# Attention with top-32 and a feed-forward block on one core: early queries and keys loaded ahead into idle tiles

## The chip, the cores and the metric

The kernel runs on one core of one Trainium2 chip. The metric is the device time of one execution in microseconds (us). Three executions of the kernel before took 791.53, 792.13 and 792.80 us; the median is 792.13 us.

## The reference

```python
# q, k, v: [4, 8, 576, 64] f32; w_in [512, 2048]; w_out [2048, 512]
scores = (q @ k^T) / 8
kth    = np.partition(scores, -32, axis=-1)[..., -32]       # 32nd largest of each row
scores = np.where(scores >= kth, scores, -1e9)
attn   = exp(scores - max) / (sum + 1e-9)
x      = (attn @ v), heads laid side by side -> [2304, 512]
h      = x @ w_in
g      = h * tanh(softplus(h))                              # mish
y      = g @ w_out                                          # [2304, 512]
```

## The kernel before

**Tiling.** Two heads are a pair, so a batch has four pairs (`PPB`), and the keys of four pairs are held at a time in `k_hi` and `k_lo`. The work runs in 72 duos. A duo `s` is two score tiles of 128 queries by 576 keys. Four duos make a block of 128 rows of `x`, so there are 18 blocks, and each block goes on through the feed-forward part. The first four duos use pairs 0, 1, 2 and 3 in turn.

**Precision.** The score product is made from three passes of reduced-precision matmuls. Keys and queries are split into a high half, written by ScalarE (ACT) as a copy (`split_k` L405, `split_q` L412), and a low half, written by GpSimd (POOL) as raw minus high (L560, L566). `w_out` is split in the same way in eight chunks (ACT L416, POOL L571).

**Stages of a duo.** TensorE (PE) makes the scores (L298) in the one PSUM buffer `ps_s`. ACT copies them to `x_sb` (L423). VectorE (DVE) finds the top 32 of each row with four MAX8 and three MATCH_REPLACE8 (L533, L540, L548). POOL takes the threshold and the negated maximum from it (`negate`, L587 and L589), ACT makes a penalty (L431), POOL subtracts it (`exponents`, L596), ACT exponentiates with a row sum (L439), POOL adds 1e-9 to the sum (`guard`, L600), DVE inverts it (`inverse`, L523), POOL multiplies (`normalise`, L607), PE transposes (L316), ACT copies (L448), PE multiplies by the values (L341 and L334). Blocks then go through `up` (L357), Mish, and `down` (L370).

**Order.** Each engine has one program written out by hand, and it works in that order; loads are issued by SyncE (SP) in its own order. At step `s` of the loop ACT does, in order: copy of the transposed tile of `s-3`, penalties of `s-1`, query split of `s+3`, feed-forward copies, score copies of `s+2`, exponentials of `s-1`, key splits due at `s`, `w_out` splits due at `s` (chunks 0 and 1 at step 0). POOL does at step `s`: `negate(s-1)`, the feed-forward split, `w_out` low parts due at `s-1` (chunks 0 and 1 at step 1), `normalise(s-2)`, `exponents(s-1)`, low query part of `s+3`, `guard(s-1)`, low key parts due at `s`. The key splits of pairs 2 and 3 are due at steps -1 and 0. DVE does `topk(s)` for one duo after another. In `topk(s)` the first MAX8 waits for `negmax_ready` of duo `s-2`, since there are two lists (`LISTS = 2`); and after the first pair of MATCH_REPLACE8 it does `inverse(s-2)`, which waits for `guard(s-2)`.

**Raw tiles.** `k_raw` has two places and `q_raw` one. SP therefore waits, before the query load of duo `s`, for the low query part of duo `s-1` (L219), and before the key load of pair `g` for the low part of pair `g-2` (L213). SP's order before the loop is: keys 0, queries 0, keys 1, `w_out` chunks 0 and 1, queries 1, keys 2, keys 3, four value loads, queries 2, four loads of `w_in` of 1 MB each; queries 3 come first in the loop. `y_sb` is written for the first time by the feed-forward output at step 15, and the third place of `p_sb` by the penalties of duo 2.

Of the kernel before, what the change touches and what calls it, by code (L numbers as in the profile page):

```python
# [5 lines left out]
F32 = mybir.dt.float32  # L6
F32R = mybir.dt.float32r
ALU = mybir.AluOpType
ACT = mybir.ActivationFunctionType

P = 128
# [4 lines left out]
PAIRS, PPB = B * H // 2, H // 2  # L16
# [12 lines left out]
DUOS = BLOCKS * PPB  # L29
# [5 lines left out]
RAWS, QS = 2, 2  # L35
XS, PS_, TS, LISTS = 4, 3, 4, 2
# [32 lines left out]
def q_cols(s):  # L69
    return 2 * P if is_mixed(s // PPB) else P  # L70


FIRST_USE, LAST_USE = {}, {}
# [26 lines left out]
                _uses.append((_g, _w, _s, _s))  # L100


def w_chunks_at(s):
    return [c for c in range(WCHUNKS) if max(c - 1, 0) == s]

# [5 lines left out]
def program(nc, k_in, q_in, v, w_in, w_out, y_out):  # L111
    with ExitStack() as ctx:
# [6 lines left out]
        def sem(name):  # L119
            return ctx.enter_context(nc.semaphore(name))  # L120

        k_raw = sb("k_raw", [P, RAWS, S])
        k_hi = sb("k_hi", [P, PPB, S], F32R)
# [29 lines left out]
        ps_y = ps("ps_y", [P, DM])  # L153

        k_loaded = [sem(f"k_loaded{i}") for i in range(RAWS)]
        q_loaded = sem("q_loaded")
        v_loaded = [sem(f"v_loaded{i}") for i in range(PPB)]
        win_loaded = sem("win_loaded")
# [3 lines left out]
        ident_zero = sem("ident_zero")  # L162
        ident_ready = sem("ident_ready")
        khi_ready = sem("khi_ready")
        klo_ready = sem("klo_ready")
        qhi_ready = sem("qhi_ready")
        qlo_ready = sem("qlo_ready")
# [34 lines left out]
        def w_part(w, c):  # L202
            return w[:, FPW * c:FPW * c + FPW, :].rearrange("p f n -> p (f n)")

        block = ctx.enter_context(nc.Block())

        @block.sync
        def _(sp):
            def load_k(g):

                if g >= RAWS:
                    sp.wait_ge(klo_ready, g - RAWS + 1)
                sp.dma_start(k_raw[:, g % RAWS, :], k_in[g, :, :]).then_inc(k_loaded[g % RAWS], 16)  # L213

            def load_q(s):
                if s >= 1:
                    sp.wait_ge(qlo_ready, s)
                n = q_cols(s)
                sp.dma_start(q_raw[:, 0:n], q_in[s, :, 0:n]).then_inc(q_loaded, 16)  # L219

            def load_w(c):
                if c >= 2:
                    sp.wait_ge(wlo_ready, c - 1)
                rows = w_out[P * FPW * c:P * FPW * c + P * FPW, :].rearrange("(t p) n -> p t n", p=P)
                sp.dma_start(w_stage(c).rearrange("p (t n) -> p t n", t=FPW), rows).then_inc(wout_loaded[c % 2], 16)

            def load_v(pr, i):
                g, layout, _, _ = V_USES[pr][i]
                if i >= 1:

                    sp.wait_ge(out_ready, V_USES[pr][i - 1][3] + 1)
                sp.dma_start(v_sb[:, pr, :, :], v[g, layout, :, :].rearrange("p (k c) -> p k c", k=KV)
                             ).then_inc(v_loaded[pr], 16)

            def store(m):
                sp.wait_ge(y_copied, m + 1)
                if is_mixed(m):
                    for h in range(2):
                        t = S * (2 * (m // BPP) + h) + MIX_START
                        sp.dma_start(y_out[t:t + D, :], y_sb[D * h:D * h + D, :]).then_inc(y_stored, 16)  # L240
                else:
                    t = S * batch_of(m) + T_START[unit_of(m)]
                    sp.dma_start(y_out[t:t + P, :], y_sb[:, :]).then_inc(y_stored, 16)

            load_k(0)
            load_q(0)
            load_k(1)
            load_w(0)
            load_w(1)
            load_q(1)  # L250
            load_k(2)
            load_k(3)
            for pr in range(PPB):
                load_v(pr, 0)
            load_q(2)
            for k in range(KC):
                sp.dma_start(win[:, k, :], w_in[P * k:P * k + P, :]).then_inc(win_loaded, 16)
            for s in range(DUOS + DOWN_SLOT):
                if 3 <= s + 3 < DUOS:
                    load_q(s + 3)  # L260
                for c in w_chunks_at(s - 1):
                    if c + 2 < WCHUNKS:
                        load_w(c + 2)
                if s == 1:
                    load_k(PPB)
                    load_k(PPB + 1)
                for g in splits_at(s - 1):
                    if PPB <= g and g + RAWS < PAIRS:
                        load_k(g + RAWS)
                for pr in range(PPB):  # L270
                    for i in range(1, len(V_USES[pr])):
                        if values_slot(V_USES[pr][i - 1][3]) == s:
                            load_v(pr, i)
                m, j = divmod(s - DOWN_SLOT, GROUPS)
                if j == GROUPS - 1 and 0 <= m < BLOCKS:
                    store(m)
            sp.wait_ge(y_stored, 16 * stores(BLOCKS - 1))

        @block.tensor
        def _(pe):  # L280
            def scores(s):
                tiles = tiles_of(s)
                last = max(g for g, _, _ in tiles)
                if s == FIRST_USE[last]:
                    pe.wait_ge(klo_ready, last + 1)
                pe.wait_ge(qlo_ready, s + 1)
                for q, k in ((q_hi, k_hi), (q_hi, k_lo), (q_lo, k_hi)):
                    first, final = q is q_hi and k is k_hi, q is q_lo
                    for h in range(2):
                        for t, (g, rows, c) in enumerate(tiles):  # L290
                            if first and h == 0 and t == 0 and s >= LAG_PT + 2:

                                pe.wait_ge(pT_copied, 2 * (s - LAG_PT - 2) + 2)
                            elif first and h == 0 and 1 <= s < LAG_PT + 2:

                                pe.wait_ge(x_copied, 2 * (s - 1) + t + 1)
                            r = slice(0, P) if rows is None else slice(D * rows, D * rows + D)
                            mm = pe.matmul(ps_s[:, t, h, 0:HALF], q[r, s % QS, c:c + P],  # L298
                                           k[r, g % PPB, HALF * h:HALF * h + HALF],
                                           start=first, stop=final, skip_group_check=True)  # L300
                            if final and h == 1:
                                mm.then_inc(scores_ready, 1)
# [95 lines left out]
        @block.scalar  # L398
        def _(act):
            def split_k(g):  # L400
                act.wait_ge(k_loaded[g % RAWS], 16 * (g // RAWS) + 16)
                if g >= PPB:

                    act.wait_ge(scores_ready, 2 * LAST_USE[g - PPB] + 2)
                act.activation(k_hi[:, g % PPB, :], k_raw[:, g % RAWS, :], ACT.Copy).then_inc(khi_ready, 1)  # L405

            def split_q(s):
                act.wait_ge(q_loaded, 16 * s + 16)
                if s >= QS:
                    act.wait_ge(scores_ready, 2 * (s - QS) + 2)  # L410
                n = q_cols(s)
                act.activation(q_hi[:, s % QS, 0:n], q_raw[:, 0:n], ACT.Copy).then_inc(qhi_ready, 1)  # L412

            def split_w(c):
                act.wait_ge(wout_loaded[c % 2], 16 * (c // 2) + 16)
# [9 lines left out]

            def penalties(s):
                act.wait_ge(limit_ready, s + 1)
                for t in range(2):
                    if s >= PS_ and t == 0:
                        act.wait_ge(pT_ready, 2 * (s - PS_) + 2)  # L430
                    act.activation(p_sb[:, s % PS_, t, :], x_sb[:, s % XS, t, :], ACT.Relu,  # L431
                                   bias=limit[:, s % TS, t:t + 1], scale=-BLOW_UP).then_inc(penalty_ready, 1)
# [87 lines left out]
        def _(dve):  # L520
# [4 lines left out]
            def topk(s):  # L525
# [8 lines left out]
                for r in range(TOPK // EIGHT - 1):  # L534
# [11 lines left out]
                    for t in range(2):  # L546
                        dve.wait_ge(found, 12 * s + 4 * r + 1 + t)
                        dve.max(best[:, t, EIGHT * r + EIGHT:EIGHT * r + 2 * EIGHT],  # L548
                                left[:, t, :]).then_inc(found, 1)

            for s in range(DUOS):
                topk(s)
            for s in range(DUOS - LAG_NORM, DUOS):
# [3 lines left out]
        def _(pool):  # L557
            def split_k(g):
                pool.wait_ge(khi_ready, g + 1)
                pool.tensor_tensor(k_lo[:, g % PPB, :], k_raw[:, g % RAWS, :], k_hi[:, g % PPB, :].bitcast(F32),  # L560
                                   ALU.subtract).then_inc(klo_ready, 1)

            def split_q(s):
                pool.wait_ge(qhi_ready, s + 1)
                n = q_cols(s)
                pool.tensor_tensor(q_lo[:, s % QS, 0:n], q_raw[:, 0:n], q_hi[:, s % QS, 0:n].bitcast(F32),  # L566
                                   ALU.subtract).then_inc(qlo_ready, 1)

            def split_w(c):
# [33 lines left out]
            def normalise(s):  # L603
                pool.wait_ge(recip_ready, s + 1)
                for t in range(2):
# [5 lines left out]
            pool.wait_ge(ident_zero, 1)  # L611
            pool.affine_select(out=ident[:, :], in_=ident[:, :], compare_op=ALU.not_equal, fill=1.0, base=0,
                               pattern=[[-1, P]], channel_multiplier=1).then_inc(ident_ready, 1)
            split_k(0)
            split_q(0)
            split_k(1)
            for s in range(-2, DUOS + LAG_NORM):
# [60 lines left out]
```

## Time and profile before

| | |
|---|---|
| median of three executions | 792.13 us |
| the profiled execution | 792.04 us |
| its span, first to last instruction | 790.2 us |
| PE busy | 718.3 us (91%) |
| DVE busy | 699.6 us (89%) |
| ACT busy | 545.8 us (69%) |
| POOL busy | 547.6 us (69%) |
| mean granted TensorE clock | 0.987 |

The span leaves out 1.8 us of the execution that lie around it. A time in a row is counted from the start of the span. An engine's idle time stands in square brackets behind an instruction, with what ended it. "x2" means that two instructions of one kind are merged in one row.

### The profile page before, as it was taken

The page shows a single profiled execution, that of the slowest core. Times are in us where ns is not written, and L with a number is a line of the kernel's source. Part 1 is how long each engine was busy: PE and PEld are TensorE (multiplying, and loading weights), DVE is VectorE, ACT ScalarE, POOL GpSimd, SP SyncE. Part 2 cuts the span into 40 slices and gives each one's busy share as a digit, 9 for nine tenths or more (in the row PEclk, how much of TensorE's full clock was granted, in tenths as well). Part 3 has the DMA queues.
Part 4 walks back from the last instruction along what each step waited for, and adds up shares of the span by engine and source line. Part 5 has one row for each costly group of instructions (what it writes and reads, how often), then busy time and mean ns, then how long its engine had stood idle before and what let it go on. Part 6 is the DMA issues. An engine that isn't in the chain of part 4 may idle for free.

```text
span 790.2 us, 16743 instructions
## 1 busy us (share of the span) xinstructions
PE 718.3 (91%) x6280; PEld 642.4 (81%) x6280; DVE 699.6 (89%) x1512; ACT 545.8 (69%) x994; POOL 547.6 (69%) x678
## 2 busy tenths in 40 slices
PE   2255777999999999999999999999999999999998
PEld 1244766888888888888888888888888888888896
DVE  4699999988999999999999999998999999997000
ACT  3477667686878786869686868686878686857420
POOL 3598658678676776787676767687767777767333
PEclk9997998999999999999999999999999999999999
DMA  8521000022122000111110000011122000000000
GB/s 297 196 63 61 8 7 8 15 58 71 53 76 88 8 21 9 37 38 37 41 54 9 22 8 21 15 58 41 54 75 89 8 21 9 21 1 15 2 14 27
DMA packets 22737, 34.64 MB, mean 44 GB/s; under 512 B 2432, under 2 KB 11648, under 8 KB 22144
## 3 DMA queue, kind: packets, MB, share of 16 engines
q1 hardware_dynamic: 22656, 33.56, 13.3%
q8 instruction: 50, 0.82, 0.4%
q14 instruction: 31, 0.25, 0.1%
HBM read 28.84 MB, written 4.72 MB: 42 GB/s over the span
## 4 chain that ended last, share of the span: by engine, by line
PE 54%; DVE 31%; POOL 6%; ACT 4%; issue 4%; DMA 1%; ACTq 0%; POOLq 0%
PE ps_u L357 21%; PE ps_y L370 16%; DVE left L540 15%; DVE top L548 12%; PE ps_s L298 5%; PE ps_s L316 5%; PE ps_o L341 5%; DVE top L533 4%; POOL p_sb L596 2%; PE ps_o L334 1%; ACT p_sb L439 1%; POOL g_lo L582 1%; POOL k_lo L560 1%; ACT pT L448 1%; POOL p_sb L607 1%
## 5 line engine op out<-in xcount | busy, mean ns | idle before, releaser
L548 DVE MAX8 top<-left 128x8 f32<-128x576 f32 x432 | 304.4, 747 | 0.0
L357 PE MATMUL ps_u<-xT,win 128*128 128x128 f32 x2304 | 277.3, 279 | 2.6 <-ACT xT L456 2.6
L357 PEld LDWEIGHTS ps_u<-xT,win 128*128 128x128 f32 x2304 | 265.5, 193 | 13.1 <-issue 9.4
L540 DVE MATCH_REPLACE8 left<-top,left 128x576 f32<-128x576 f32 x288 | 212.0, 745 | 0.0
L596 POOL TENSOR_TENSOR p_sb<-x_sb,p_sb 128x576 f32<-128x576 f32 x144 | 200.7, 1416 | 0.0
L439 ACT ACTIVATE p_sb<-p_sb,neg_max 128x576 f32<-128x576 f32 x144 | 111.2, 775 | 61.5 <-POOL p_sb L596 60.8
L607 POOL TENSOR_SCALAR p_sb<-p_sb,recip 128x576 f32<-128x576 f32 x144 | 106.1, 747 | 50.8 <-DVE recip L523 50.8
L370 PE MATMUL ps_y<-w_hi,g_hi 128*128 128x512 f32 x288 | 119.0, 413 | 0.7 <-ACT y_sb L479 0.7
L423 ACT ACTIVATE x_sb<-ps_s 128x576 f32<-128x576 f32 x144 | 85.6, 648 | 42.5 <-PE ps_s L298 42.4
L370 PE MATMUL ps_y<-w_hi,g_lo 128*128 128x512 f32 x288 | 113.0, 392 | 0.0
L370 PE MATMUL ps_y<-w_lo,g_hi 128*128 128x512 f32 x288 | 112.3, 390 | 0.0
L533 DVE MAX8 top<-x_sb 128x8 f32<-128x576 f32 x144 | 101.2, 745 | 10.7 <-ACT x_sb L423 10.1
L431 ACT ACTIVATE p_sb<-x_sb,limit 128x576 f32<-128x576 f32 x144 | 103.4, 770 | 8.2 <-POOL limit L587 8.2
L540 DVE MATCH_REPLACE8 left<-top,x_sb 128x576 f32<-128x576 f32 x144 | 106.0, 744 | 0.0
L448 ACT ACTIVATE pT<-ps_s 128x512 f32<-128x512 f32 (+1 forms) x144 | 84.6, 638 | 24.0 <-PE ps_s L316 24.0
L316 PE MATMUL ps_s<-ident,p_sb 128*128 128x128 f32 x648 | 85.7, 279 | 8.0 <-POOL p_sb L607 5.5
L298 PE MATMUL ps_s<-k_hi,q_hi 64*128 64x288 f32 (+1 forms) x288 | 43.4, 361 | 52.3 <-ACT pT L448 22.1
L582 POOL TENSOR_TENSOR g_lo<-g_raw,g_hi 128x1024 fp32r<-128x1024 f32 x36 | 86.0, 2389 | 3.1
L341 PEld LDWEIGHTS ps_o<-pT,v_sb 128*64 128x64 f32 x1280 | 70.8, 139 | 17.1 <-issue 14.0
L341 PE MATMUL ps_o<-pT,v_sb 128*64 128x128 f32 x1280 | 79.4, 279 | 5.4 <-ACT pT L448 5.4
L298 PEld LDWEIGHTS ps_s<-k_hi,q_hi 64*128 64x128 f32 (+1 forms) x288 | 25.7, 198 | 70.7 <-issue 47.4
L316 PEld LDWEIGHTS ps_s<-ident,p_sb 128*128 128x128 f32 x648 | 75.3, 144 | 9.4 <-ACT x_sb L423 5.3
(36 smaller groups left out, 729.9 us busy)
## 6 DMA issues: line engine op xcount, KB each, us to landing
v_sb<-v_in SPq DMA_DIRECT2D x32, 320.0 KB, 3.6
k_raw<-k_in SPq DMA_DIRECT2D x16, 288.0 KB, 2.9
q_raw<-q_in SPq DMA_DIRECT2D x64, 64.0 KB, 1.8
g_raw<-w_out SPq DMA_DIRECT2D x8, 512.0 KB, 3.7
win<-w_in SPq DMA_DIRECT2D x4, 1024.0 KB, 10.0
y_out<-y_sb SPq DMA_DIRECT2D x16, 256.0 KB, 2.0
q_raw<-q_in SPq DMA_DIRECT2D x8, 128.0 KB, 2.1
y_out<-y_sb SPq DMA_DIRECT2D x4, 128.0 KB, 2.5
```

The source lines that it names most:

```text
L298: mm = pe.matmul(ps_s[:, t, h, 0:HALF], q[r, s % QS, c:c + P], k[r, g % PPB, HALF * h:HALF * h + HALF], start=first, stop=final, skip_grou ...
L316: mm = pe.transpose(flat[:, P * k:P * k + P], p[:, P * k:P * k + P], ident[:, :])
L341: mm = pe.matmul(ps_o[D * h:D * h + D, j, :], v_sb[:, j, k, D * h:D * h + D], pT[:, s % 2, SPLIT_AT * h + k, :], start=(k == 0), stop=(k = ...
L357: mm = pe.matmul(ps_u[:, n % 2, i, :], win[:, k, P * f:P * f + P], xT[:, k, :], start=(k == 0), stop=(k == KC - 1), skip_group_check=True)
L370: mm = pe.matmul(ps_y[:, :], g[:, f, :], w[:, f, :], start=(f == 0 and g is g_hi and w is w_hi), stop=(f == FT - 1 and g is g_lo), skip_gr ...
L431: act.activation(p_sb[:, s % PS_, t, :], x_sb[:, s % XS, t, :], ACT.Relu, bias=limit[:, s % TS, t:t + 1], scale=-BLOW_UP).then_inc(penalty ...
L439: act.activation(p, p, ACT.Exp, bias=neg_max[:, s % TS, t:t + 1], scale=SCALE, accum_out=denom[:, s % TS, t:t + 1]).then_inc(exp_ready, 1)
L533: dve.max(best[:, t, 0:EIGHT], x[t]).then_inc(top8_ready, 1)
L540: dve.match_replace(out=left[:, t, :], in_to_replace=best[:, t, EIGHT * r:EIGHT * r + EIGHT], in_values=x[t] if r == 0 else left[:, t, :], ...
L548: dve.max(best[:, t, EIGHT * r + EIGHT:EIGHT * r + 2 * EIGHT], left[:, t, :]).then_inc(found, 1)
L596: pool.tensor_tensor(p, x_sb[:, s % XS, t, :], p, ALU.subtract).then_inc(arg_ready, 1)
L607: pool.tensor_scalar(p, p, recip[:, s % TS, t:t + 1], 1.0, ALU.mult, ALU.mult).then_inc(p_ready, 1)
```

## The change

The queries of duos 0 to 3 are loaded by one DMA into `y_sb` (512 columns, 128 for each duo). The keys of pairs 2 and 3 are loaded into the two halves of the third place of `p_sb`. Neither load waits. Both stand, with the keys of pairs 0 and 1, ahead of the `w_out` loads in SP's order. `q_raw` is first used by duo 4 and `k_raw` again by pairs 4 and 5, whose loads move from step 1 of SP's loop to before the `w_in` loads. The low half of pair 0's keys is made by DVE ahead of its first top-k, and no longer by POOL. Penalties of duo 2 gain a wait for the low part of pair 3.

```diff
+STAGED = PPB
...
+        def k_source(g):
+            return p_sb[:, PS_ - 1, g - RAWS, :] if RAWS <= g < PPB else k_raw[:, g % RAWS, :]
+
+        def q_source(s):
+            return y_sb[:, P * s:P * s + P] if s < STAGED else q_raw[:, 0:q_cols(s)]
...
             def load_k(g):
-                if g >= RAWS:
-                    sp.wait_ge(klo_ready, g - RAWS + 1)
+                if g == PPB:
+                    sp.wait_ge(klo0_ready, 1)
+                elif g > PPB:
+                    sp.wait_ge(klo_ready, 1 if g == PPB + 1 else g - RAWS)
...
             def load_q(s):
-                if s >= 1:
+                if s > STAGED:
                     sp.wait_ge(qlo_ready, s)
...
             load_k(0)
-            load_q(0)
+            sp.dma_start(y_sb[:, :].rearrange("p (s c) -> p s c", s=STAGED),
+                         q_in[0:STAGED, :, 0:P].rearrange("s p c -> p s c")).then_inc(q_staged, 16)
             load_k(1)
+            for g in range(RAWS, PPB):
+                sp.dma_start(k_source(g), k_in[g, :, :]).then_inc(k_staged[g - RAWS], 16)
             load_w(0)
             load_w(1)
-            load_q(1)
-            load_k(2)
-            load_k(3)
+            load_q(STAGED)
             for pr in range(PPB):
                 load_v(pr, 0)
-            load_q(2)
+            load_k(PPB)
+            load_k(PPB + 1)
...
-                if 3 <= s + 3 < DUOS:
+                if STAGED < s + 3 < DUOS:
                     load_q(s + 3)
...
-                if s == 1:
-                    load_k(PPB)
-                    load_k(PPB + 1)
...
             def scores(s):                                      # PE
-                if s == FIRST_USE[last]:
-                    pe.wait_ge(klo_ready, last + 1)
+                if s == 0:
+                    pe.wait_ge(klo0_ready, 1)
+                elif s == FIRST_USE[last]:
+                    pe.wait_ge(klo_ready, last)
...
             def penalties(s):                                   # ACT
                 act.wait_ge(limit_ready, s + 1)
+                if s == PS_ - 1:
+
+                    act.wait_ge(klo_ready, PPB - 1)
...
+            dve.wait_ge(khi_ready, 1)                           # DVE, ahead of topk(0)
+            dve.tensor_tensor(k_lo[:, 0, :], k_raw[:, 0, :], k_hi[:, 0, :].bitcast(F32),
+                              ALU.subtract).then_inc(klo0_ready, 1)
             for s in range(DUOS):
                 topk(s)
...
-            split_k(0)                                          # POOL
             split_q(0)
             split_k(1)
```

The splits on ACT and POOL read `k_source(g)` and `q_source(s)` in place of the raw tiles, and wait for `k_staged` and `q_staged` where the data is staged.

## Rows read from the trace of the kernel before

**Rows 1.** The page: busy time of the engines, and the last chain by engine.

```profile
PE 718.3 (91%) x6280; PEld 642.4 (81%) x6280; DVE 699.6 (89%) x1512; ACT 545.8 (69%) x994; POOL 547.6 (69%) x678
...
PE 54%; DVE 31%; POOL 6%; ACT 4%; issue 4%; DMA 1%; ACTq 0%; POOLq 0%
```

**Rows 2.** Chain that ended last: start us, us, what; from 100 us on.

```profile
113.65 0.23 POOL limit L587
...
127.98 5.29 PE ps_u L357 x32
...
140.34 3.77 PE ps_u L357 x32
...
352.94 1.31 DVE top L533 x2
...
362.64 1.31 DVE top L533 x2
```

**Rows 3.** Waits of DVE over the span: engine, line, releaser: us, times, longest.

```profile
DVE recip L523 <- POOL denom L600: 25.7, 8, 9.3
DVE top L533 <- ACT x_sb L423: 10.1, 1, 10.1
DVE top L533 <- POOL neg_max L589: 0.6, 1, 0.6
```

**Rows 4.** Timeline to 12 us: start us, us, engine line, op, [idle before <-releaser].

```profile
3.68 0.68 ACT L405 ACTIVATE k_hi<-k_raw 128x576 fp32r<-128x576 f32 x1 [1.68 <-DMA k_raw<-k_in]
...
4.45 1.40 POOL L560 TENSOR_TENSOR k_lo<-k_raw,k_hi 128x576 fp32r<-128x576 f32 x1 [2.99 <-ACT k_hi L405]
5.21 0.68 ACT L405 ACTIVATE k_hi<-k_raw 128x576 fp32r<-128x576 f32 x1 [0.64 <-DMA k_raw<-k_in]
5.80 0.46 POOL L566 TENSOR_TENSOR q_lo<-q_raw,q_hi 128x128 fp32r<-128x128 f32 x1
...
6.40 0.85 PE L298 MATMUL ps_s<-k_hi,q_hi 64*128 64x288 f32 x4 [6.40 <-POOL q_lo L566]
...
7.50 0.71 PE L298 MATMUL ps_s<-k_hi,q_lo 64*128 64x288 f32 x4
...
9.18 0.31 ACT L412 ACTIVATE q_hi<-q_raw 128x128 fp32r<-128x128 f32 x1 [3.29 <-DMA q_raw<-q_in]
9.39 1.17 ACT L423 ACTIVATE x_sb<-ps_s 128x576 f32<-128x576 f32 x2
9.56 0.45 POOL L566 TENSOR_TENSOR q_lo<-q_raw,q_hi 128x128 fp32r<-128x128 f32 x1 [1.94 <-ACT q_hi L412]
...
10.06 1.42 DVE L533 MAX8 top<-x_sb 128x8 f32<-128x576 f32 x2 [10.06 <-ACT x_sb L423]
```

**Rows 5.** Timeline from 15 to 40 us, same columns.

```profile
19.72 1.40 DVE L533 MAX8 top<-x_sb 128x8 f32<-128x576 f32 x2
...
27.83 2.00 ACT L416 ACTIVATE w_hi<-g_raw 128x1024 fp32r<-128x1024 f32 x2
28.02 1.41 POOL L560 TENSOR_TENSOR k_lo<-k_raw,k_hi 128x576 fp32r<-128x576 f32 x1 [1.19 <-ACT k_hi L405]
...
29.52 0.23 POOL L587 TENSOR_SCALAR limit<-top 128x2 f32<-128x2 f32 x1
...
30.08 1.42 DVE L533 MAX8 top<-x_sb 128x8 f32<-128x576 f32 x2 [0.64 <-POOL neg_max L589]
...
38.62 0.17 DVE L523 RECIPROCAL recip<-denom 128x2 f32<-128x2 f32 x1 [5.68 <-POOL denom L600]
```

**Rows 6.** Stretches: busy us of each engine, granted clock, DMA share, GB/s.

```profile
10.00:20.00 10.00, 2.83 (x16) 2.32 (x18) 9.94 (x21) 2.52 (x6) 1.87 (x3) 1.00 0.99 370
...
125.00:130.00 5.00, 3.83 (x22) 3.58 (x23) 5.00 (x12) 4.23 (x8) 4.91 (x5) 0.50 0.01 3
```

**Rows 7.** The page: a DVE group of instructions: busy, mean ns, idle before.

```profile
L540 DVE MATCH_REPLACE8 left<-top,left 128x576 f32<-128x576 f32 x288 | 212.0, 745 | 0.0
```

More of the change, by code:

```diff
@@ L155, in program @@
         k_loaded = [sem(f"k_loaded{i}") for i in range(RAWS)]
+        k_staged = [sem(f"k_staged{i}") for i in range(PPB - RAWS)]
+        q_staged = sem("q_staged")
         q_loaded = sem("q_loaded")
@@ L164, in program @@
         khi_ready = sem("khi_ready")
+        klo0_ready = sem("klo0_ready")
         klo_ready = sem("klo_ready")
@@ L400, in split_k @@
             def split_k(g):
-                act.wait_ge(k_loaded[g % RAWS], 16 * (g // RAWS) + 16)
+                if RAWS <= g < PPB:
+                    act.wait_ge(k_staged[g - RAWS], 16)
+                else:
+                    act.wait_ge(k_loaded[g % RAWS], 16 if g < RAWS else 16 * (g // RAWS))
                 if g >= PPB:
                     act.wait_ge(scores_ready, 2 * LAST_USE[g - PPB] + 2)
-                act.activation(k_hi[:, g % PPB, :], k_raw[:, g % RAWS, :], ACT.Copy).then_inc(khi_ready, 1)
+                act.activation(k_hi[:, g % PPB, :], k_source(g), ACT.Copy).then_inc(khi_ready, 1)
             def split_q(s):
-                act.wait_ge(q_loaded, 16 * s + 16)
+                if s < STAGED:
+                    act.wait_ge(q_staged, 16)
+                else:
+                    act.wait_ge(q_loaded, 16 * (s - STAGED) + 16)
                 if s >= QS:
@@ L411, in split_q @@
                 n = q_cols(s)
-                act.activation(q_hi[:, s % QS, 0:n], q_raw[:, 0:n], ACT.Copy).then_inc(qhi_ready, 1)
+                act.activation(q_hi[:, s % QS, 0:n], q_source(s), ACT.Copy).then_inc(qhi_ready, 1)
             def split_w(c):
@@ L559, in split_k @@
                 pool.wait_ge(khi_ready, g + 1)
-                pool.tensor_tensor(k_lo[:, g % PPB, :], k_raw[:, g % RAWS, :], k_hi[:, g % PPB, :].bitcast(F32),
+                pool.tensor_tensor(k_lo[:, g % PPB, :], k_source(g), k_hi[:, g % PPB, :].bitcast(F32),
                                    ALU.subtract).then_inc(klo_ready, 1)
@@ L565, in split_q @@
                 n = q_cols(s)
-                pool.tensor_tensor(q_lo[:, s % QS, 0:n], q_raw[:, 0:n], q_hi[:, s % QS, 0:n].bitcast(F32),
+                pool.tensor_tensor(q_lo[:, s % QS, 0:n], q_source(s), q_hi[:, s % QS, 0:n].bitcast(F32),
                                    ALU.subtract).then_inc(qlo_ready, 1)
```

## The prediction

> **What bounds the kernel now.** I read the page first. TensorE is busy for 91% of the span and DVE for 89%, and the last chain lies on PE for 54% and on DVE for 31% [rows 1]. So neither engine alone sets the end, and the question is where the chain lies on which. The chain in order of time answers it: from 10.06 us it runs along DVE's top-k instructions without a break but for one excursion at 30 to 38 us, until 113.65 us, where it leaves DVE for POOL's threshold; it then goes by ACT to PE, which holds it with `up` groups of 3.77 us [rows 2]. Later it comes back to DVE: two successive first MAX8 stand at 352.94 and 362.64 us [rows 2], so a duo costs DVE 9.70 us when nothing holds it. At the end it is PE again.
>
> The first 113 us are thus DVE's alone, and PE's later work is behind DVE by data and by the order of the programs. What the changed part can give is DVE's idle time ahead of that point. The waits of DVE list it: 10.1 us for the first score copy, 0.6 us for a negated maximum, and 25.7 us in eight waits of the reciprocal for `guard` [rows 3]. Of these eight, the first is 5.68 us long, in front of the reciprocal at 38.62 us [rows 5]; the other seven lie behind the change's reach.
>
> **Why those waits are there.** The timeline shows three things. (a) The first scores run from 6.40 us and their last group ends at 7.50 + 0.71 = 8.21 us, but ACT copies them only at 9.39 us, because the query split of duo 1 stands ahead of the copy in ACT's order and waited 3.29 us for a load that was issued only when POOL had freed `q_raw` [rows 4]. (b) Each next query load goes into the same DMA queue behind whatever was issued before it, and the queue is full: 370 GB/s at a DMA share of 0.99 from 10 to 20 us [rows 6]. ACT's in-order program puts the key splits of pairs 2 and 3 behind those query splits, so the low part of pair 3 is made at 28.02 us, although POOL waited for nothing but ACT's part of it [rows 5]. `negate(0)` on POOL stands behind it and starts at 29.52, though duo 0's top-k was over when DVE began duo 1 at 19.72 [rows 5]. (c) ACT's two `w_out` splits stand behind the same instructions (27.83), and everything of duo 0 from `negate(0)` to `guard(0)` follows; DVE gets it at 38.62, 9.10 us after `negate(0)` began [rows 5].
>
> **The change part by part.**
>
> *The staged query load.* Before, 64 KB of queries and 288 KB of keys landed between ACT's wait ends at 3.68 and 5.21 us: 352 KB in 1.53 us, 230 KB a us [rows 4]. By bytes the four duos' 256 KB land 256 / 230 = 1.11 us after the first keys, at 3.66 + 1.11 = 4.77 us, and pair 1's keys 192 / 230 = 0.83 us later than before, at 6.02. If the cost were by row pieces (128 of the query load and 128 of the key load in 1.53 us, so 167 a us, and 512 pieces now), they would land at 3.66 + 3.07 = 6.7 us. By the full queue's 370 KB a us [rows 6] it would be 3.66 + 0.69 = 4.35. I take 4.77, since the pieces of 512 bytes were in the measured 1.53 us too, and keep 4.35 and 6.7 as ends.
>
> The Trainium skill has a rule for such a load: in "DMA: Bandwidth & Descriptors", section "Anatomy of one DMA", a fit made on the other DMA path gives about 2.0 us fixed plus the bytes at 436 GB/s. From the issue at 1.17 us plus 0.4 us of issuing, that estimate is a landing at 4.2 us, and the sum below would be about 0.5 us larger. The page's table asks for at least 512 bytes a piece for full rate, and these pieces have exactly 512; no row here shows smaller ones.
>
> *From the queries to the first scores.* A landing seen at 9.15 us led to ACT's split at 9.18, POOL's low part at 9.56 for 0.45, done at 10.01; and PE starts 0.14 us after POOL's low part ends (5.80 + 0.46 against 6.40) [rows 4]. So PE starts L + 1.00 = 5.77 us, where it was 6.40.
>
> *Pair 0's low keys on DVE.* It leaves POOL: 1.40 us, which stood ahead of the low queries [rows 4]. On DVE it starts at the same 4.45. The trace shows no tensor_tensor on DVE. The nearest row is a 576-column MATCH_REPLACE8 at 0.745 us [rows 7], done at 5.20; the upper end is POOL's own 1.40, done at 5.85, which would put PE 0.2 us later than the queries do (5.85 + 0.14 = 5.99); below 0.745 nothing is gained, as the queries come later. DVE has nothing to do then, so it costs DVE nothing. I take 0.745. If this cover were gone it would be paid once, 0.75 us.
>
> The Trainium skill gives the price in "VectorE: DVE Perf Modes", section on the TRN2 errata: (N + 151) / 0.96 ns for a 4-byte tensor_tensor. For 576 columns that estimate is 0.76 us; the sum does not change by it.
>
> *The first copy.* ACT makes the key split of pair 1 at 6.05 to 6.73 and the query split of duo 1 (already there) by 7.05, ahead of the scores' end at 5.77 + 1.81 = 7.58. The copy follows at once, and DVE starts 10.06 - 9.39 = 0.67 us after the copy does [rows 4], with 0.02 for the signal: 8.27 us. **Gain 10.06 - 8.27 = 1.79 us.** With the ends of L it is 2.2 and about -0.1.
>
> *The 0.64 and 5.68 us waits.* Followed by the same durations: pair 1's low keys on POOL 6.8 to 8.2, duo 1's queries to 8.65, scores(1) 8.75 to 10.6, its copies to 11.8, pair 2's high part to 12.45, low part to 13.95, scores(2) to 15.85, copies to 17.05, pair 3's high part to 17.7, low part to 19.2, both `w_out` high parts to 19.6. Each is now limited by the work itself; the loads are there. DVE ends duo 0 at 8.27 + 9.66 = 17.93, so `negate(0)` starts at 19.2 and is 1.3 us late. It isn't waited for: duo 2's first MAX8 is due at 8.27 + 2 x 9.66 = 27.6. **Gain 0.64.** `guard(0)` comes 9.1 us after `negate(0)`, at 28.3. The reciprocal is due at 27.6 + 2.86 (MAX8 twice and MATCH_REPLACE8 twice) = 30.5. It is 2.2 us early. **Gain 5.68.** The next reciprocal has a duo's 9.70 us more to come, and POOL isn't as far behind, so nothing is late next on DVE until the chain leaves it.
>
> *The moved loads.* 192 + 576 KB now go ahead of the `w_out` chunks. Ahead of and with both chunks the queue then has 2432 KB; at 230 to 370 KB a us the last chunk lands at 10 to 13 us, before ACT wants it at 17.7. Keys 4 and 5 (576 KB) go ahead of `w_in`, which is used at step 6, after 60 us. SP's added waits (pair 0's and pair 1's low keys, at 5.2 and 8.2 us) hold the `w_in` issue behind them until 8.2 us, while the queue still has work: nothing. Chunks 2 and 3 of `w_out` were issued after POOL's low parts; they now stand behind `w_in` and land at about 28 us, when ACT comes to them after the exponentials of duo 0. The wait of the penalties of duo 2 is for something done at 19.2 us: nothing.
>
> **The sum.** 1.79 + 0.64 + 5.68 = 8.11 us on DVE. Behind 113 us nothing is changed, and all of PE's and POOL's work waits in the end for DVE's results, so the whole moves by as much. Against the profiled execution, 792.04 - 8.11 = 783.9 us; its median is 0.09 higher, so I predict **784.0 us**. Ends of the unknown costs: 8.5 by the fast load (783.6), 6.2 by the slow one (785.9).
>
> **The rivals.**
>
> *The staged load is slow (785.9 us).* The piece count decides and L is 6.7. For it: 512 pieces in one load is more than any load of the start has. Against it: nothing waits for those pieces by name in the timeline. Only the 6.3 us of the two later waits are won.
>
> *A part of the 5.68 us stays (786 us).* The cover is 2.2 us. If `w_out` or pair 3 comes 4 us later than I have it, about 2 us of the wait are left. For it: ACT and POOL have long in-order queues here. Against: all of those loads are issued by 8 us.
>
> *The clock falls elsewhere (782.5 or 785.5 us).* From 125 to 130 us the granted clock was 0.50, the lower level of 1.2 GHz, after PE had been idle for much of the time before, and an `up` group took 5.29 us where it takes 3.77 at 2.4 GHz [rows 2, 6]: 1.5 us, on the chain. When everything comes 8 us earlier, this stretch may be missing or a second one may fall on PE's part of the chain. Each is worth 1.5 us. The skill's "TensorE: Matmul & The Clock Gate", Part 1, says that the default is the throttled state and that idleness brings it back; by that rule the trace agrees, with its 0.50 stretch. PE's waiting pattern behind 40 us stays as it is by my account, so I keep the forecast.
>
> *PE holds the end (792 us).* PE is busy for 718.3 us [rows 1], and the end is its own. If its work were not held by DVE, an earlier DVE would only wait later. Against it: only 72 us of PE's span are idle, most of them ahead of 113 us, where the chain is DVE's.
>
> *Slower: the `w_out` chunks come too late.* Place: ACT's split of chunk 1, which stands ahead of the penalties of duo 0. From the start of these splits at 27.83 to the reciprocal at 38.62 are 10.8 us [rows 5]. If the chunk that is now behind 768 KB more landed later than about 28 us, the reciprocal would be as late as before, and the early start would be lost in the same wait; each us beyond costs one: at 31 us, 795 us. Against it: that takes 2432 KB at under 90 KB a us.
>
> **How the numbers follow.** Chances: the forecast (783 to 785 us) 0.58; slow staged load 0.12; part of the wait stays 0.08; clock 0.14, half each way; PE holds the end 0.04; slower 0.04. A measurement tells about 0.2%, 1.6 us, from no change. Faster is all but the last two: 0.92; same 0.04; slower 0.04. The range leaves out the last two and some of the edges: 781.8 to 786.8 us.
>
> **What would show it.** Right: DVE's first MAX8 at about 8.3 us; no DVE idle time from there to past 100 us; PE's first matmul at 5.8 and ACT's copy at 7.6; `negate(0)` at about 19.2 and the first reciprocal at about 30.5, not waited for; duo 6's MAX8 8.1 us earlier than before, and the same shift at the `up` groups behind 140 us and at the end. Wrong: a first copy that still waits for queries, L above 5 us, a reciprocal that waits for `guard(0)`, or a shift that shrinks between 113 and 200 us; the last would mean that PE, ACT or POOL there isn't held by DVE.

## The result, and the profile after

Four executions of the changed kernel took 782.78 to 784.48 us, median **783.81 us**; the kernel before took 792.46 us in the median of four in the same comparison. The ratio is 0.9889, with a 95% interval of 0.9871 to 0.9907: faster by 8.65 us, where the forecast was 8.1 us and 784.0. The profiled execution took 782.78 us with a span of 781.0 us, the fastest of the four.

The page of the changed kernel, busy time and chain, stands against [rows 1]: busy times are as they were, only the span is shorter.

```profile
PE 717.6 (92%) x6280; PEld 641.7 (82%) x6280; DVE 700.3 (90%) x1513; ACT 546.1 (70%) x994; POOL 546.3 (70%) x677
...
PE 55%; DVE 32%; POOL 4%; ACT 4%; issue 4%; DMA 1%; SPq 0%; ACTq 0%; POOLq 0%
```

The waits of DVE in the changed kernel (engine, line, releaser: us in total, times, longest) answer to [rows 3]. What went is to be seen line by line: one reciprocal fewer waits, the 0.6 us for the negated maximum has gone, and what was 10.1 us ahead of the first MAX8 is now a wait of 4.2, an instruction of 0.76, and a wait of 3.0.

```profile
DVE recip L548 <- POOL denom L628: 19.2, 7, 9.3
DVE k_lo L577 <- ACT k_hi L424: 4.2, 1, 4.2
DVE top L558 <- ACT x_sb L445: 3.0, 1, 3.0
```

The timeline of the changed kernel to 31 us answers to [rows 4] and [rows 5].

```profile
3.52 0.68 ACT L424 ACTIVATE k_hi<-k_raw 128x576 fp32r<-128x576 f32 x1 [1.52 <-DMA k_raw<-k_in]
...
4.24 0.76 DVE L577 TENSOR_TENSOR k_lo<-k_raw,k_hi 128x576 fp32r<-128x576 f32 x1 [4.24 <-ACT k_hi L424]
4.26 0.31 ACT L434 ACTIVATE q_hi<-y_sb 128x128 fp32r<-128x128 f32 x1
4.66 0.65 POOL L594 TENSOR_TENSOR q_lo<-y_sb,q_hi 128x128 fp32r<-128x128 f32 x1 [3.20 <-ACT q_hi L434]
...
5.45 0.85 PE L314 MATMUL ps_s<-k_hi,q_hi 64*128 64x288 f32 x4 [5.45 <-POOL q_lo L594]
...
6.57 0.68 ACT L424 ACTIVATE k_hi<-k_raw 128x576 fp32r<-128x576 f32 x1 [2.00 <-DMA k_raw<-k_in]
...
7.36 1.17 ACT L445 ACTIVATE x_sb<-ps_s 128x576 f32<-128x576 f32 x2
...
8.02 1.42 DVE L558 MAX8 top<-x_sb 128x8 f32<-128x576 f32 x2 [3.03 <-ACT x_sb L445]
...
19.53 0.23 POOL L615 TENSOR_SCALAR limit<-top 128x2 f32<-128x2 f32 x1
...
28.41 0.22 POOL L628 TENSOR_SCALAR denom<-denom 128x2 f32<-128x2 f32 x1 [0.58 <-ACT p_sb L464]
...
30.09 0.15 DVE L548 RECIPROCAL recip<-denom 128x2 f32<-128x2 f32 x1
```

DVE starts at 8.02 in place of 10.06 us, and from there to 167 us it has no idle bracket: the first reciprocal stands at 30.09, 1.5 us after `guard(0)` ended.

The chain of the changed kernel from 100 us on (start us, us, what) answers to [rows 2].

```profile
105.12 0.23 POOL limit L615
...
117.62 1.66 PE ps_s L314 x12
119.29 4.71 PE ps_u L373 x32
...
131.06 3.77 PE ps_u L373 x32
```

This gives two marks. The threshold of duo 9 comes at 105.12 in place of 113.65 us: 8.53 us are won by then. From there to the end of the span the changed kernel takes 781.0 - 105.12 = 675.9 us, the one before 790.2 - 113.65 = 676.6. The other 0.7 us of this profile is in the `up` group of 4.71 us, where it was 5.29, and in the scores in front of it, which took 1.66 us and in the kernel before 1.81:

```profile
126.17 1.81 PE ps_s L298 x12
```

Further on the shift holds. The first MAX8 of duo 6 moved from 74.67 to 66.14 us (8.5), the `up` group behind from 140.34 to 131.06 (9.3), and the end of the span by 9.2.

The stretches of the changed kernel around the `up` group of 4.71 us (busy us of PE, PEld, DVE, ACT, POOL, granted clock, DMA share, GB/s) show PE nearly idle, and then the clock down for a part of the next stretch, as in [rows 6]:

```profile
112.00:117.00 5.00, 0.86 (x8) 0.62 (x6) 5.00 (x11) 4.75 (x7) 2.65 (x7) 1.00 0.05 15
117.00:122.00 5.00, 4.38 (x28) 4.13 (x29) 5.00 (x12) 3.77 (x8) 5.00 (x5) 0.66 0.01 3
```

### The profile page after: what moved, and what is told of

Read it like the earlier page. It is cut to its first block, busy times and chain, and to the rows that moved or that the text cites. A ratio compares the mean times of both kernels' runs of the same rounds, so it can differ in the third digit from the quotient of the medians.

```text
span 781.0 us, 16741 instructions
## 1 busy us (share of the span) xinstructions
PE 717.6 (92%) x6280; PEld 641.7 (82%) x6280; DVE 700.3 (90%) x1513; ACT 546.1 (70%) x994; POOL 546.3 (70%) x677
## 4 chain that ended last, share of the span: by engine, by line
PE 55%; DVE 32%; POOL 4%; ACT 4%; issue 4%; DMA 1%; SPq 0%; ACTq 0%; POOLq 0%
PE ps_u L373 22%; PE ps_y L386 16%; DVE left L565 15%; DVE top L573 12%; PE ps_s L314 5%; PE ps_s L332 5%; PE ps_o L357 5%; DVE top L558 5%; POOL p_sb L624 1%; PE ps_o L350 1%; ACT p_sb L464 1%; POOL g_lo L610 1%; ACT pT L473 1%; POOL p_sb L635 1%; POOL k_lo L588 1%
## 5 line engine op out<-in xcount | busy, mean ns | idle before, releaser
L332 PEld LDWEIGHTS ps_s<-ident,p_sb 128*128 128x128 f32 x648 | 75.2, 144 | 10.4 <-ACT x_sb L445 5.9
```

The source lines that it names most:

```text
L332: mm = pe.transpose(flat[:, P * k:P * k + P], p[:, P * k:P * k + P], ident[:, :])
```

## The experiments

The theory was that all of the gain is idle time of DVE ahead of 113 us, that the serial query loads caused nearly all of it, and that it is passed on one for one. The rivals were that the late keys of pairs 2 and 3 did it, and that PE holds the end. Each kernel was timed beside the kernel before, in three comparisons: e1 to e4, e5 to e7, e8 to e10. The changed kernel itself was not timed again in them. The median of the kernel before was 792.05, 792.51 and 792.43 us there, against 792.46 beside the changed kernel, so a difference of less than about 0.4 us between two comparisons says nothing.

**e1, the low half of pair 0's keys back on POOL.**

```diff
-            dve.wait_ge(khi_ready, 1)
-            dve.tensor_tensor(k_lo[:, 0, :], ...).then_inc(klo0_ready, 1)
...
+            pool.wait_ge(khi_ready, 1)                # ahead of split_q(0)
+            pool.tensor_tensor(k_lo[:, 0, :], ...).then_inc(klo0_ready, 1)
```

> The changed kernel with one part undone: the low half of pair 0's keys is made by POOL ahead of the low queries again. My theory (the start of DVE is shifted through to the end, one for one): POOL makes these keys from 4.25 to 5.65 us and the low queries to 6.1, PE starts at 6.25 in place of 5.45, DVE's first MAX8 at 8.8 in place of 8.0, the reciprocal still doesn't wait, and the time is 0.8 us above the changed kernel, about 784.6 us. Rival (this part is hidden behind the load of the queries or behind ACT's order): first MAX8 at 8.0 and 783.8 us.

Measured: 784.79 us, 1.0 above the changed kernel; ratio to before 0.9907 (0.9892 to 0.9922). The first MAX8 stands at 9.04 us, and the reciprocal doesn't wait. This part is worth about 1.0 us, and 1.02 against e3 of the same comparison, by the start of DVE alone.

**e2, keys staged, queries serial.**

```diff
-            return y_sb[:, P * s:P * s + P] if s < STAGED else q_raw[:, 0:q_cols(s)]
+            return q_raw[:, 0:q_cols(s)]
...
-                if s > STAGED:
+                if s >= 1:
                     sp.wait_ge(qlo_ready, s)
```

The query loads also go back to their old places, queries 0 behind keys 0, queries 1 behind the two `w_out` chunks, which now stand behind all four key loads, and queries 2 behind the values.

> The changed kernel with the queries loaded one duo at a time through the one raw tile, as before; the keys stay staged. My theory (the serial query loads hold everything): queries 1 are now behind both early w_out chunks and two key loads and land at 10 to 11 us, so DVE starts at 11 to 12; queries 3 land behind w_in at about 26 us, the split of pair 3 stands behind them in order, and the wait of the first reciprocal comes back with 5 to 6 us. Time 791 to 794 us, no gain over the kernel before. Rival (the late keys 2 and 3 made the wait of the reciprocal): the wait is gone, time about 786 us.

Measured: 794.02 us, ratio 1.0020 (1.0011 to 1.0030): slower than before by 0.2%, at the upper end of the 791 to 794 expected. The timeline of this kernel shows why: the three query splits wait for their loads.

```profile
11.01 0.31 ACT L431 ACTIVATE q_hi<-q_raw 128x128 fp32r<-128x128 f32 x1 [4.90 <-DMA q_raw<-q_in]
...
14.51 0.31 ACT L431 ACTIVATE q_hi<-q_raw 128x128 fp32r<-128x128 f32 x1 [2.11 <-DMA q_raw<-q_in]
...
28.08 0.31 ACT L431 ACTIVATE q_hi<-q_raw 128x128 fp32r<-128x128 f32 x1 [11.61 <-DMA q_raw<-q_in]
```

Its first reciprocal waits 5.69 us again. Keys loaded earlier are worth nothing while the queries come one by one, and they push the second query load back: DVE starts at 11.89 us.

**e3, queries staged, keys of pairs 2 and 3 through `k_raw`.**

```diff
-            return p_sb[:, PS_ - 1, g - RAWS, :] if RAWS <= g < PPB else k_raw[:, g % RAWS, :]
+            return k_raw[:, g % RAWS, :]
...
+            load_k(2)                                 # behind w_out chunks 0 and 1
+            load_k(3)
             load_q(STAGED)
```

The loads of pairs 4 and 5 go back to step 1 of SP's loop too, so the moved loads are undone with the staged keys.

> The changed kernel with the queries staged, and the keys of pairs 2 and 3 loaded through the two raw places as before, behind the w_out chunks. My theory: they land at 10 to 12 us, ACT wants them at 12.1 and 17.3, so nothing is late: first MAX8 at 8.0, no wait of a reciprocal before 100 us, 783.8 us, same as the changed kernel within 0.5. Rival (both parts are needed): pair 3 is late, part of the 5.68 us stays, 786 us or more.

Measured: 783.77 us, ratio 0.9894 (0.9881 to 0.9908), the same as the changed kernel. DVE starts at 8.22 us and no reciprocal waits before 100 us. ACT's key splits of pairs 2 and 3 stand at 11.52 and 16.65 us there and wait for no load. So neither the staged keys nor the moved loads of pairs 4 and 5 are worth anything that shows here; the queries carry the gain, with the 1.0 us of e1.

**e4, a measured delay at DVE's start.** Eight subtractions that nothing uses, ahead of `topk(0)`.

```diff
+                    for i in range(8):
+                        dve.tensor_tensor(left[:, i % 2, :], x_sb[:, s % XS, i % 2, :], x_sb[:, s % XS, i % 2, :],
+                                          ALU.subtract).then_inc(spare, 1)
```

> The changed kernel with eight subtractions of 576 columns on DVE that nothing uses, ahead of its first top-k: some 5.8 us more of DVE. My theory (time at the start of DVE is passed on one for one): 783.8 + 5.8 = 789.6 us, and every landmark behind is later by the same amount. Rival (PE holds the end, the early stage has slack): less than 2 us more, 784 to 786 us.

Measured: 791.53 us, 7.7 above the changed kernel. The size in the expectation was wrong, the law was right: the eight took 7.33 us, and the first MAX8 moved from 8.02 to 15.97, 7.95 us; the span grew by 8.0. The other 0.6 us is that the block waits for both score copies, where the first MAX8 waits for one. The timeline rows of this kernel:

```profile
8.61 7.33 DVE L588 TENSOR_TENSOR left<-x_sb 128x576 f32<-128x576 f32 x8 [3.49 <-ACT x_sb L446]
15.97 1.42 DVE L559 MAX8 top<-x_sb 128x8 f32<-128x576 f32 x2
```

**e5, the same eight ahead of duo 24,** where the chain of the kernel before lies on PE. The edit is the same, at `s == 24`.

> The changed kernel with the same eight unused subtractions (about 5.8 us of DVE) ahead of the top-k of duo 24, in the stretch where the last chain lies on PE. If PE alone holds that stretch and DVE runs ahead of it with room, the time stays at 783.8 to 785 us. If DVE is the pace there too (9.70 us a duo against 9.68 on PE, so no room is ever made), all of it comes through: 789.6 us. I hold that PE trails DVE by a fixed order with a few us of room, so that about half is lost: 786 to 788 us.

Measured: 792.05 us, 8.2 above the changed kernel. My expectation of half was wrong, and so was the rival that PE has the stretch for itself. The block took 8.65 us of DVE, and nearly all of it came through:

```profile
245.75 8.65 DVE L588 TENSOR_TENSOR left<-x_sb 128x576 f32<-128x576 f32 x8
254.43 1.42 DVE L559 MAX8 top<-x_sb 128x8 f32<-128x576 f32 x2
```

PE idled behind the block (3.3 us in one wait for POOL's `normalise`), and the granted clock of this kernel fell to 0.52 between 260 and 265 us. DVE's waits for `guard` add up to 18.5 us in this kernel, against 19.2 in the changed one, so only 0.7 of the 8.65 us was made up for by shorter waits. How long those waits would have been without the lower clock is not separated.

**e6, the key splits of pairs 2 and 3 one step earlier** on ACT and POOL.

```diff
-SPLIT_SLOT = {g: g - 3 if g < PPB else LAST_USE[g - PPB] - 2 for g in range(PAIRS)}
+SPLIT_SLOT = {g: g - 4 if g < PPB else LAST_USE[g - PPB] - 2 for g in range(PAIRS)}
...
-                if s > -2:                            # on ACT and on POOL
-                    for g in splits_at(s):
-                        split_k(g)
+                for g in splits_at(s):
+                    split_k(g)
```

> The changed kernel with the key splits of pairs 2 and 3 one step earlier in ACT's and POOL's order. My theory (only the waits of DVE count, and there is none left before 100 us): POOL takes duo 0's threshold at 17.7 in place of 19.5 us, the sum of duo 0 is ready more than 3 us ahead of the reciprocal, and the time doesn't move: 783.8 us, within 0.4. Rival (an earlier POOL carries through): up to 1.8 us less, 782 us.

Measured: 783.79 us, ratio 0.9893 (0.9880 to 0.9907): no change. `guard(0)` comes at 26.96 us, and the reciprocal at 30.32 is now 3.1 us behind its end. More room where nothing waits is worth nothing.

**e7, the first scores start earlier.** On e6:

```diff
+                if s == 0:                            # PE; low parts are waited for before their pass
+                    pe.wait_ge(khi_ready, 1)
+                    pe.wait_ge(qhi_ready, 1)
...
+                    if s == 0 and k is k_lo:
+                        pe.wait_ge(klo0_ready, 1)
+                    if s == 0 and final:
+                        pe.wait_ge(qlo_ready, 1)
...
             split_q(0)                                # ACT
+            split_q(1)
+            copy_x(0)
             split_k(1)
...
             split_q(0)                                # POOL
+            split_q(1)
             split_k(1)
```

> As the kernel with the key splits one step earlier, and: PE's first scores begin with the high halves and wait for the low keys and the low queries only before the passes that use them; ACT splits duo 1's queries and copies duo 0's scores before it splits pair 1's keys. My theory: PE starts at 4.7 in place of 5.45 us, its last pass is held by the low queries at 5.4 to 5.9, the copy begins at 6.5, DVE's first MAX8 stands at 7.15 in place of 8.02, no reciprocal waits before 100 us, and the time falls by the same 0.9: 782.9 us. Rival (the clock or PE absorbs it): 783.8 us.

Measured: 783.24 us, ratio 0.9885 (0.9872 to 0.9899). The first MAX8 stands at 7.33 us, 0.9 ahead of e6's 8.25, but the time fell by 0.55. The forecast of 782.9 was 0.3 us short. The profile of this kernel has a longer `up` group behind the idle stretch than any but e3's, which is the next question:

```profile
104.42 0.24 POOL limit L622
...
118.74 5.66 PE ps_u L379 x32
```

**e8, e9 and e10, PE kept busy.** Matmuls whose result is never read, at step 11 between the transposes and the scores; e8 is on e7, e9 on the changed kernel, e10 has eight of them also at each of steps 6 to 10.

```diff
+            def idle_work(n):
+                for _ in range(n):
+                    pe.matmul(ps_y[:, :], k_hi[:, 0, 0:P], k_hi[:, 0, 0:DM], start=True, stop=True,
+                              skip_group_check=True)
...
+                if s == DOWN_SLOT - 1:
+                    idle_work(16)
```

> The kernel with the first scores earlier (783.24 us), with 16 matmuls of 512 columns on PE at step 11, between the transposes and the scores, into a buffer that nothing has used yet; their result is never read. In the profiles so far PE idles there for 4.8 us, then the granted clock is 0.50 for 3 to 7 us and the up group behind it takes 4.7 to 5.8 us in place of 3.77. Theory (that one group at the lower level is passed on to the end): the clock stays at 1.00 there, the group takes 3.77 us and the time falls by 1.2 to 2.3 us, to 781.0 to 782.0. Rival (the group's length is made up for by slack behind it, or the clock falls anyway): 783.2 us, or more where the added matmuls delay the scores.

> The changed kernel as it is (783.81 us) with the same 16 matmuls at step 11. By the same theory the time falls by the same 1.2 to 2.3 us, to 781.5 to 782.6; with the kernel above it tells whether the earlier first scores are worth their 0.9 us when the clock doesn't blur it. Rival: 783.8 us.

> As the first of these, with 8 such matmuls also at each of steps 6 to 10. Theory: the lower clock of those steps never reached the end, because DVE sets the pace there, so nothing more is won: the same time as with step 11 alone, within 0.4 us. Rival (PE's catching up in those steps matters): up to 1 us less, or some more where the added work delays the values.

Measured: e8 **780.79 us**, ratio 0.9856 (0.9839 to 0.9872); e9 781.59 us, 0.9865 (0.9850 to 0.9880); e10 780.84 us, 0.9856 (0.9842 to 0.9871). The stretches and the chain of e8:

```profile
112.00:117.00 5.00, 3.89 (x19) 2.89 (x19) 5.00 (x11) 4.97 (x8) 2.81 (x5) 1.00 0.04 13
117.00:122.00 5.00, 5.00 (x49) 4.83 (x50) 5.00 (x12) 3.74 (x7) 5.00 (x5) 1.00 0.01 3
```

```profile
104.33 0.23 POOL limit L629
...
117.94 3.77 PE ps_u L379 x32
```

Against e7 (the same kernel without them) e8 is 2.5 us faster, a little above the 1.2 to 2.3 that I expected. e9 against the changed kernel is 2.2 us faster. e8 against e9 is 0.80 us, which is the earlier first scores with the clock out of the way (first MAX8 at 7.24 against 8.18). e10 adds nothing, so the lower clock of steps 6 to 10 costs nothing. And the spread of four times shrinks: 0.24 us for e8 against 0.67 for e7, and 0.12 for e9 against 1.70 for the changed kernel.

The marks of the profiles without a delay, together: DVE's first MAX8, the threshold of duo 9, the length of the `up` group at step 11, the span behind the threshold, and DVE's waits for `guard` behind the threshold. (In e9 that `up` group isn't on the last chain; its row in the timeline is as long as e8's.)

| kernel | first MAX8 | threshold | `up` group | rest of span | waits for `guard` in it |
|---|---|---|---|---|---|
| before | 10.06 | 113.65 | 5.29 | 676.6 | 20.0 |
| changed | 8.02 | 105.12 | 4.71 | 675.9 | 19.2 |
| e1 | 9.04 | 106.12 | 5.14 | 676.5 | 19.9 |
| e2 | 11.89 | 115.77 | 5.22 | 676.6 | 19.9 |
| e3 | 8.22 | 105.31 | 5.83 | 677.2 | 20.5 |
| e6 | 8.25 | 105.35 | 5.10 | 676.6 | 20.0 |
| e7 | 7.33 | 104.42 | 5.66 | 677.1 | 20.5 |
| e8 | 7.24 | 104.33 | 3.77 | 674.6 | 17.9 |
| e9 | 8.18 | 105.28 | 3.8 | 674.5 | 17.9 |
| e10 | 7.34 | 104.43 | 3.77 | 674.6 | 17.9 |

The threshold follows the first MAX8 by 97.1 us in every kernel in which no reciprocal waits before it, and by 103.6 and 103.9 in the two that have the early waits. The rest of the span follows the `up` group: from e8 to e7 the group is 1.9 us longer, the scores in front of it 0.7 (1.8 us for 1.07), and the rest of the span 2.5.

The last column shows the way that this takes. The rest of the span less DVE's waits for `guard` is 656.6 or 656.7 us in all ten kernels (up to the rounding), so what the slow group costs PE is found again, whole, in DVE's waits behind it. In e7 the first of them is 2.6 us long, at 167.93 us; e8 has none there. The row of e7, and then the waits over the span of e7 and of e8 (us in total, times, longest):

```profile
167.93 0.17 DVE L555 RECIPROCAL recip<-denom 128x2 f32<-128x2 f32 x1 [2.61 <-POOL denom L635]
...
DVE recip L555 <- POOL denom L635: 20.5, 7, 9.3
...
DVE recip L562 <- POOL denom L642: 17.9, 6, 9.3
```

## Why the prediction was right

*What bounds.* Right for the part that counted: DVE's idle time ahead of 113 us was nearly the whole gain, passed on one for one (8.5 of the 9.2 us of the profile; e1 and e4 for the passing on). It was 8.53 us at duo 9 and at duo 6, 0.2 more than the brackets that went (2.04 + 0.64 + 5.68 = 8.36). That PE "holds" the stretches where the chain names it was left as a reading of the chain; e5 shows that a delay on DVE there comes through nearly whole too. And e8 and e9 show the other half: 1.4 to 2.5 us less of PE behind 113 us come through as well. At 9.70 us a duo on DVE and a PE that is as full, neither had room for the other in these runs. None of the signs of being wrong came: the shift grew from 8.5 us at 113 us to 9.3 at 131, by the clock, and did not shrink.

*The number.* That the median came within 0.2 us of the forecast is partly luck. The four executions spread over 1.7 us, and the kernel before took 792.46 us beside them where the forecast counted from 792.13; the gain was 8.65 us, 0.5 more than forecast.

*The staged load.* Mis-sized, harmlessly. I took a landing at 4.77 us from 230 KB a us. ACT's split of these queries began at 4.26, and the chain of e4 has the load from 1.17 for 3.27 us, so at 4.44:

```profile
1.17 3.27 DMA y_sb<-q_in
```

In the other kernels whose chain has this load it landed at 4.27 to 4.55 us. That is about the 4.35 of the fast end, 0.2 to 0.5 us ahead of my value, and well off the 6.7 by pieces. The Trainium skill's fit in "DMA: Bandwidth & Descriptors", "Anatomy of one DMA", gave an estimate of 4.2, nearer than mine: the traces have 4.27 to 4.55.

*Pair 0's low keys on DVE.* 0.76 us, against 0.745 taken; the formula of "VectorE: DVE Perf Modes" in the Trainium skill had 0.76. What I had at nothing wasn't quite: beside it POOL's low queries took 0.65 us and not 0.45. So PE started at 5.45, 0.3 earlier than forecast, where the load alone would have given more.

*The start.* 2.04 us were won in the profile, 1.79 forecast. Part of the difference is the run: the start-up of e3, e5, e6 and e9 is the same but for the later loads, and their first MAX8 stands at 8.13 to 8.25, 1.8 to 1.9 us ahead of the kernel before; the changed kernel's profile has the earliest first keys of all (3.52 against 3.71 to 3.83). Pair 1's keys landed later than I had them (6.55 for 6.02), so ACT's splits ended at 7.45 and the copy began at 7.36, 0.1 us after the scores' end. That cover had 0.5 us in my sum and none in this profile; in e6, whose keys landed by 5.66, it held.

*The 0.64 and 5.68 us.* Both gone. `negate(0)` at 19.53 (19.2 forecast), the reciprocal at 30.09 (30.5). The room of 2.2 us was 1.5. e2 and e3 together bear out the reason (b) of the prediction: the low part of pair 3 was late because its split stands behind the query splits in ACT's order, not because of its own load. What the prediction didn't say is that the staged keys could then be left out altogether.

*The moved loads.* Nothing, as forecast (e3 undoes them at no cost), and the rival of late `w_out` chunks had no part in it: ACT split them at 17.85 without a wait.

*The clock.* A rival at 1.5 us each way. The stretch stayed, shorter, and its share in the profile was 0.7 us, not a case of its own but a noise on every time. This term was mis-sized: its full price is 2.2 to 2.5 us in the medians (e9, e8), more than I had for the one group, because the lower clock lasts through the scores in front of it too and its `up` group can be longer than the 5.29 us of [rows 2] (5.83 in e3). In the changed kernel's profile, the fastest of its four runs, it was 1.4 us (675.9 against 674.5).

## What to carry to other kernels

Look for the engine that, once started, doesn't stop until another takes over the pace: here DVE's idle time ahead of that point was worth its full length. A wait in the start-up can come from a single raw tile that makes small loads queue behind large ones. Staging into tiles that are idle until later cost nothing here, but stage what stands first in the in-order program: here the queries, not the keys. And where PE idles shortly before the chain passes to it, try a few unused matmuls: here 16 of them, 3.9 us in an idle stretch of 4.8, won 2.2 to 2.5 us. The best version here is e8, at 780.79 us.

## What the runs showed of the hardware that I had not expected

- In these traces subtractions of two tensors on DVE and POOL's instructions slow each other. One of 576 columns took 0.76 us on DVE at the start; eight in a row beside a busy POOL took 8.65 us in e5, and the last of them alone 2.9 us, beside POOL's subtraction of 1024 columns (2.75 us, where 2.4 is its mean). In e4 the three of the eight that ran while POOL was idle (10.4 to 12.5 us) took 0.74 each. In e5's block POOL's add of 2 columns (`guard`) took 0.73 us, where it takes 0.22. The rows of POOL in e5:

```profile
247.39 0.73 POOL L639 TENSOR_SCALAR denom<-denom 128x2 f32<-128x2 f32 x1 [1.30 <-ACT p_sb L465]
248.21 0.59 POOL L626 TENSOR_SCALAR limit<-top 128x2 f32<-128x2 f32 x1
...
251.03 2.75 POOL L621 TENSOR_TENSOR g_lo<-g_raw,g_hi 128x1024 fp32r<-128x1024 f32 x1
```

DVE's MAX8 and MATCH_REPLACE8, which run beside POOL all the time, show nothing of this: 0.75 us each in the mean.

- The granted clock reads 1.00 in the first 40 us of every profile, but twelve score matmuls take 1.8 us there, as long as at 0.50, and 0.99 in the steady stretches. So the column can't be trusted for the start of a span, and the durations have to be read instead.

- Around step 11 PE was idle for 4.6 to 4.8 us, and in that stretch or just behind it the granted clock fell to 0.50 (1.2 GHz) in every profile of a kernel without the added matmuls there; with them it stayed at 1.00 (e8, e9, e10). The `up` group behind it took 4.71 to 5.83 us, with no change near it in the code, and four times of one kernel spread over 0.6 to 1.7 us. That this variation is what goes in e8 and e9 fits their spreads of 0.24 and 0.12 us but is not shown: the single runs behind the others' spreads were not traced one by one.
